# An expert stage of 25 planned tiles: idle tiles placed as second tiles of the first experts

## The reference

```
attn = softmax(window-64 causal scores of q, k) @ v          # (4, 8, 576, 64)
x = attn as (2304, 512)
h = x @ w_in ; g = h - tanh(h) ; x = g @ w_out              # d_ff 2048
logits = unit(x) @ unit(expert_emb).T / tau                  # 8 experts
expert_idx = argmax(logits) ; gate_w = softmax(logits) at it
for e in range(8):                                           # w1[e] 512 x 1024, w2[e] 1024 x 512
    mask = expert_idx == e
    out[mask] = gate_w[mask, None] * (maximum(x[mask] @ w1[e], 0) @ w2[e])
```

## Time and profile before

| | |
|---|---|
| median of 3 runs | 871.54 us (871.42 to 874.31) |
| the profiled execution, its own time | 873.4 us |
| its span, first to last instruction | 871.6 us |
| TensorE busy in the span | 809.0 us (93%) |
| VectorE, ScalarE, GpSimd | 478.6, 360.3, 218.6 us |
| mean granted clock of TensorE | 0.967 |
| matmuls with w1, with w2 in each of their three forms | 176, 176 |
| gathers and scatters of tiles | 25, 25 |

### The profile page before, as it was taken

The page is one execution under the profiler, slowest core; times in us unless marked ns, Lnnn a source line. Parts: engine busy times, 40 slices in busy tenths (PEclk is TensorE's granted clock), DMA queues, the critical chain, the costliest instruction groups (busy, mean ns, idle before and its releaser), DMA issues. The chain is left out here.

```text
span 871.6 us, 16504 instructions
## 1 busy us (share of the span) xinstructions
PE 809.0 (93%) x4604; PEld 689.5 (79%) x4605; DVE 478.6 (55%) x1421; ACT 360.3 (41%) x880; POOL 218.6 (25%) x284
## 2 busy tenths in 40 slices
PE   6699999999999999999999999399999999999992
PEld 5588888888888888888888998277888888888871
DVE  7356655775577557755774575555534252545422
ACT  4444554333433343334332223416544253655423
POOL 4647542223222322231223001221111111111111
PEclk9699999999999999999999999679999999999996
DMA  9862113331322133313216120126452342565110
GB/s 176 243 202 64 45 37 97 74 71 36 96 71 72 37 93 75 73 37 97 55 38 211 51 65 1 39 83 235 170 198 83 132 143 73 199 228 218 51 40 22
DMA packets 106310, 87.87 MB, mean 101 GB/s; under 512 B 79012, under 2 KB 80169, under 8 KB 106242
## 3 DMA queue, kind: packets, MB, share of 16 engines
q1 hardware_dynamic: 98386, 74.92, 29.4%
q0 software_dynamic: 4624, 11.32, 4.2%
q10 hardware_dynamic: 3232, 0.79, 0.5%
HBM read 152.87 MB, written 11.46 MB: 189 GB/s over the span
## 5 line engine op out<-in xcount | busy, mean ns | idle before, releaser
L1233 PE MATMUL banks<-xh,win_h 128*128 128x384 f32 x384 | 137.8, 359 | 2.1 <-POOL xl L529 2.1
L1235 PE MATMUL banks<-xh,win_l 128*128 128x384 f32 x384 | 130.8, 341 | 0.0
L1234 PE MATMUL banks<-xl,win_h 128*128 128x384 f32 x384 | 130.5, 340 | 0.0
L701 ACT ACTIVATE gf<-banks 128x384 f32<-128x384 f32 x96 | 47.1, 491 | 183.0 <-PE banks L1235 182.9
L519 POOL TENSOR_TENSOR sm<-sm,rr 128x384 f32<-128x384 f32 x48 | 50.6, 1055 | 275.8 <-DVE rr L872 275.8
L1233 PE MATMUL banks<-wout_h,gh 128*128 128x512 f32 x288 | 118.8, 413 | 0.0
L1235 PE MATMUL banks<-wout_h,gl 128*128 128x512 f32 x288 | 113.7, 395 | 0.0
L1234 PE MATMUL banks<-wout_l,gh 128*128 128x512 f32 x288 | 113.2, 393 | 0.0
L933 DVE TENSOR_TENSOR gl<-gf,gh 128x384 fp32r<-128x384 f32 x96 | 55.0, 573 | 104.2 <-ACT gh L708 104.2
L708 ACT CAST gh<-gf 128x384 fp32r<-128x384 f32 x96 | 49.1, 512 | 129.5 <-PE banks L1235 128.3
L929 DVE TENSOR_TENSOR gf<-banks,gf 128x384 f32<-128x384 f32 x96 | 53.2, 554 | 69.6 <-ACT gf L701 68.5
(11 more groups left out here) (186 smaller groups left out, 1537.8 us busy)
## 6 DMA issues: line engine op xcount, KB each, us to landing
w1raw<-in_moe_w_dram SPq DMA_DIRECT2D x104, 512.0 KB
w2raw<-in_moe_w_dram SPq DMA_DIRECT2D x104, 512.0 KB
x2T<-unit_embeddings SPq DMA_DIRECT2D x20, 256.0 KB, 3.4
junk<-unit_embeddings SPq DMA_DIRECT2D x20, 256.0 KB, 3.5
x_rows<-x SPq DMA_DIRECT2D x6, 768.0 KB, 6.3
wout_raw<-in_moe_w_out_dram SPq DMA_DIRECT2D x4, 1024.0 KB, 7.7
win_raw<-in_moe_w_in_dram SPq DMA_DIRECT2D x3, 1024.0 KB, 10.1
vw<-in_v_dram SPq DMA_DIRECT2D x16, 192.0 KB, 3.4
```

Source lines behind the costliest of these rows:

```text
L701: act.activation(gf[c % 2][:], psH[c % 2], ACT.Tanh).then_inc(tanh_ready, 1)
L1233: pe.matmul(to, sh, mh, start=start, stop=False)
L1234: pe.matmul(to, sh, ml, start=False, stop=False)
L1235: return pe.matmul(to, sl, mh, start=False, stop=stop)
```

## The change

The plan is computed anew. It counts the tiles that are left over (`idle_tiles` = 25 less the sum of `tiles`), and marks as many experts from the first on (`left_over`, by comparing the expert's number, `em8` + 8, with that count). Each marked expert is `given` one tile more. `ends`, `starts` and the openings are computed from `given`. Within a marked expert the second tile is the idle one: its row in the table lies behind the expert's filled rows, and the tiles behind it move down by one (`local`, `second`, `third`). `rows` is now found for each tile by the expert whose stretch it lies in (`shown`). `is_idle` is one for the second tile of each marked expert that has tokens, and `plan[:, 3]` is one less it. So with three tiles left over, experts 0, 1 and 2 have an idle second tile, and no tile is idle behind the last expert.

The program of the four engines after the plan is the same, instruction for instruction, apart from the banks: `psY` is 4 and 5, `psXG` is 6.

```diff
--- before.py
+++ after.py
@@ -202,6 +202,10 @@
         experts_ended = sb("experts_ended", [P, NTILE], scope=phase2)
         row = [sb(f"row{i}", [P, 1], scope=phase2) for i in range(2)]
         rows = sb("rows", [P, 1], I32, phase2)
+        idle_tiles = sb("idle_tiles", [P, 1], scope=phase2)
+        total = sb("total", [P, 1], scope=phase2)
+        is_idle = sb("is_idle", [P, NTILE], scope=phase2)
+        d8 = [sb(f"d8_{i}", [P, E], scope=phase2) for i in range(12)]
 
         mstep, dstep = sem("mstep"), sem("dstep")
         ident_made, masks_made, pads_zeroed, consts_made = sem("ident_made"), sem("masks_made"), sem("pads_zeroed"), sem("consts_made")
@@ -270,8 +274,8 @@
         psJ = banks[:, 0, :]
         psG = [banks[:, i, :] for i in (0, 1)]
         psHT = [banks[:, i, :] for i in (2, 3)]
-        psY = [banks[:, i, :] for i in (4, 6)]
-        psXG = banks[:, 5, :]
+        psY = [banks[:, i, :] for i in (4, 5)]
+        psXG = banks[:, 6, :]
 
         q_blocks, k_blocks = (x.rearrange("b h (i p) d -> p (b h i) d", p=WINDOW) for x in (q, k))
         win_rows = w_in.rearrange("(k p) f -> p k f", p=P)
@@ -1058,29 +1062,52 @@
             then(dve.tensor_copy(count, psN))
             then(dve.tensor_tensor(cmp18[:], count.unsqueeze(2).broadcast_to((P, E, MAXT)), tiles18[:], ALU.is_gt))
             then(dve.tensor_reduce(tiles, cmp18[:], AX, ALU.add))
-            then(dve.tensor_tensor(prod8[:], tiles.unsqueeze(1).broadcast_to((P, E, E)), tri8[:], ALU.mult))
+            left_over, given, shown, later, second, third, local, base = (t[:] for t in d8[:8])
+            then(dve.tensor_reduce(total[:], tiles, AX, ALU.add))
+            then(dve.tensor_scalar(idle_tiles[:], total[:], -1.0, float(NTILE), ALU.mult, ALU.add))
+            then(dve.tensor_scalar(left_over, em8[:, 0, :], float(E), idle_tiles[:, 0:1], ALU.add, ALU.is_lt))
+            then(dve.tensor_tensor(given, tiles, left_over, ALU.add))
+            then(dve.tensor_tensor(prod8[:], given.unsqueeze(1).broadcast_to((P, E, E)), tri8[:], ALU.mult))
             then(dve.tensor_reduce(ends, prod8[:], AX, ALU.add))
-            then(dve.tensor_scalar(moves, tiles, -float(P), float(REGION), ALU.mult, ALU.add))
-            then(dve.tensor_scalar(passed, ends, pcol[:, 0:1], None, ALU.is_le))
-            then(dve.tensor_tensor(jumped, passed, moves, ALU.mult))
+            then(dve.tensor_tensor(starts, ends, given, ALU.subtract))
+            then(dve.tensor_scalar(local, starts, -1.0, pcol[:, 0:1], ALU.mult, ALU.add))
+            then(dve.tensor_scalar(second, local, 1.0, None, ALU.is_equal))
+            then(dve.tensor_scalar(third, local, 2.0, None, ALU.is_ge))
+            then(dve.tensor_scalar(base, tiles, -1.0, None, ALU.add))
+            then(dve.tensor_tensor(second, second, base, ALU.mult))
+            then(dve.tensor_tensor(second, second, third, ALU.subtract))
+            then(dve.tensor_tensor(second, second, left_over, ALU.mult))
+            then(dve.tensor_tensor(local, local, second, ALU.add))
+            then(dve.scalar_tensor_tensor(out=base, in0=rowbase[:, 0, :], scalar=1.0 / P, in1=local, op0=ALU.mult, op1=ALU.add))
+            then(dve.tensor_scalar(passed, ends, pcol[:, 0:1], None, ALU.is_gt))
+            then(dve.tensor_scalar(later, starts, pcol[:, 0:1], None, ALU.is_gt))
+            then(dve.tensor_tensor(shown, passed, later, ALU.subtract))
+            then(dve.tensor_tensor(jumped, shown, base, ALU.mult))
             then(dve.tensor_reduce(row[0][:], jumped, AX, ALU.add))
-            then(dve.tensor_scalar(row[1][:], row[0][:], 1.0 / P, pcol[:, 0:1], ALU.mult, ALU.add))
-            dve.tensor_scalar(rows[:], row[1][:], float(E * REGION // P), None, ALU.min).then_inc(rows_planned, 1)
+            dve.tensor_scalar(rows[:], row[0][:], float(E * REGION // P), None, ALU.min).then_inc(rows_planned, 1)
 
 
             then(dve.tensor_tensor(ended[:], jcol[:].unsqueeze(2).broadcast_to((P, NTILE, E)), ends.unsqueeze(1).broadcast_to((P, NTILE, E)), ALU.is_ge))
             then(dve.tensor_reduce(experts_ended[:], ended[:], AX, ALU.add))
             then(dve.tensor_scalar(plan[:, 0, :], experts_ended[:], float(E - 1), None, ALU.min))
-            then(dve.tensor_tensor(starts, ends, tiles, ALU.subtract))
-            then(dve.scalar_tensor_tensor(out=filled, in0=tiles, scalar=0.0, in1=notfirst[:], op0=ALU.is_gt, op1=ALU.mult))
+            then(dve.scalar_tensor_tensor(out=filled, in0=given, scalar=0.0, in1=notfirst[:], op0=ALU.is_gt, op1=ALU.mult))
             then(dve.tensor_tensor(ended[:], jcol[:].unsqueeze(2).broadcast_to((P, NTILE, E)), starts.unsqueeze(1).broadcast_to((P, NTILE, E)), ALU.is_ge))
             then(dve.tensor_tensor(moved[:], ended[:], filled.unsqueeze(1).broadcast_to((P, NTILE, E)), ALU.mult))
             then(dve.tensor_reduce(changes[:, 1:NTILE + 1], moved[:], AX, ALU.add))
+            then(dve.scalar_tensor_tensor(out=later, in0=tiles, scalar=0.0, in1=left_over, op0=ALU.is_gt, op1=ALU.mult))
+            then(dve.tensor_scalar(starts, starts, 1.0, None, ALU.add))
+            then(dve.tensor_tensor(ended[:], jcol[:].unsqueeze(2).broadcast_to((P, NTILE, E)), starts.unsqueeze(1).broadcast_to((P, NTILE, E)), ALU.is_equal))
+            then(dve.tensor_tensor(moved[:], ended[:], later.unsqueeze(1).broadcast_to((P, NTILE, E)), ALU.mult))
+            then(dve.tensor_reduce(is_idle[:], moved[:], AX, ALU.add))
             then(dve.tensor_tensor(plan[:, 1, :], changes[:, 1:NTILE + 1], changes[:, 0:NTILE], ALU.subtract))
             then(dve.tensor_copy(plan[:, 2, :], changes[:, 1:NTILE + 1]))
             then(dve.tensor_scalar(plan[:, 2, :], plan[:, 2, :], 1, None, ALU.bitwise_and))
-            then(dve.tensor_scalar(plan[:, 3, :], jcol[:], ends[:, E - 1:E], None, ALU.is_lt))
+            then(dve.tensor_scalar(plan[:, 3, :], is_idle[:], -1.0, 1.0, ALU.mult, ALU.add))
             dve.sem_inc(planned, 1)
             low_first_w1([0])
 
```

## The result

| | before | after |
|---|---|---|
| median of the runs | 872.01 us (4 runs) | 883.45 us (4 runs, 881.06 to 885.14) |
| ratio | 1 | 1.0124, 95% interval 1.0094 to 1.0155 |
| the profiled execution, its own time and span | 873.4, 871.6 us | 885.1, 883.3 us |

The change makes the kernel 1.2% slower, 11.4 us. The forecast was 872.9 us in a range of 869.3 to 878.5, so it was wrong, by 10.6 us. The step that failed is the clock of TensorE: the forecast's sum put nothing for a fall of the clock in the new pauses, and it fell three times, for 5.7 us. Waits in the same sum were also too short, by 5.0 us together, of which Part 3 had foreseen 0.6.

A forecast was written before the change was run, and what follows sets the result against it. TensorE was taken as the bound, busy 230 of 230 us at full clock through the middle of the expert stage. Terms -12.3 + 3.7 + 5.3 + 3.7 + 0.6 + 0.4 = +1.4 us gave 872.9 us, range 869.3 to 878.5.

The forecast's parts named there:

- Part 3: Weight fetches: w1 pieces for experts 1 and 2 land late, 0.3 us each, 0.6 us cost in all.
- Part 1: End of the program: idle tiles no longer follow the last real tile, and its step transposes no tokens; gain 12.3 us.
- Part 4: Plan: 18 more VectorE operations delay the copy of the token numbers and the first gather; cost 0.4 us.
- Part 5: Banks: token transposes and second products swap banks 5 and 6; nothing either way.
- these lie between what held and what fell: New TensorE pauses, 4.2 us in steps 2 and 5, 3.4 in step 1, against earlier pauses that kept or lost the clock.
- Rival A: TensorE's clock falls in the new waits; two falls of 2.2 us give 877.3 us; chance 0.15.
- Part 2: Idle tiles inside the expert stage take cover away: cost 3.7 us at expert 2, 5.3 at expert 1, 3.7 at expert 0.
- rival B: Weight fetches for the next expert: w1 pieces land 2 to 3 us later than taken in both experts, 877 us; chance 0.10.

The follow-up runs named there:

- the experiment: The kernel before with the change's banks and 18 more small plan operations, idle tiles still at the end: 872.35 us against 872.28, ratio 1.0007.
- the kernel with both edits: The changed kernel with filler matmuls in TensorE's idle-tile skips and half the bytes of w1 for experts 1 to 7: 877.12 us, ratio to before 1.0047.

## Why the prediction was wrong

**What held.** The bound and the structure: 22 runs of each kind, TensorE the bound, steps of 12.3 us outside the affected ones. Part 1: 12.3 us forecast, 11.9 at the end plus 0.5 in the last step (11.01 us from its w1 run to its hidden transposes, 11.51 in the others). Part 4: 0.4 us forecast, 0.34 by the trace, 0.2 to 0.3 in the experiment, under what runs can tell. Part 5: nothing, as forecast. The transposes of step 2, held by the casts ahead of relu, came 7.63 us behind the w1 run; 7.57 was forecast. The pause behind them was 4.2 us, as forecast, with the casts back to back.

**What failed.** The forecast's own case assumed that the clock holds, so its sum has no term for a fall. It gave that the sentence "these lie between what held and what fell" and then a chance of 0.15 to its falling. It fell in or just behind all three long pauses of the change, and cost 5.7 us in the runs themselves. The pause of 4.2 us ahead of the w1 run of tile 3 came out as forecast, and the clock fell behind it all the same. Rival A had the mechanism right and a price of 4.4 us for two falls, 2.2 each; the three cost 2.4, 1.6 and 1.6. The third is in step 1, whose pause between products was not 3.4 but 5.3 us; that 3.4 us would have held is doubtful, since a pause of 3.4 us lost the clock in the kernel with both edits. The account that rival A names from the Trainium skill ("TensorE: Matmul & The Clock Gate", HAM oscillation) describes what happened: a wait behind a burst, and a cold start of the next. The trace agrees for the three pauses of 4.2 us and more, with a granted clock of 0.50 in the run behind each, and not for those of 2.2 to 2.8 us in the same trace, which kept 1.00. I had two held pauses of a little over 2 us and one fall, 5.7 us behind the last products, to go by, and two pauses of 4.2 us between them; to take the favourable side there was a choice, not a reading.

**What was mis-sized in Part 2.** Three terms, with the change's own profile:

| term | forecast | measured | more by |
|---|---|---|---|
| step 1, token transposes to w2 run | 0.36 us | 1.83 | 1.5 |
| step 5, w1 run to hidden transposes | 7.6 (Part 3 had 0.3 beside it) | 9.5 | 2.0 |
| the other pauses around idle tiles, each 0 to 0.4 us longer | | | 1.5 together |

The first is TensorE's restart. I took 0.36 us from a step in which it goes straight on. Here it had waited for the gather, and 0.92 us of idle time stand ahead of the run, ended by nothing but "issue". That these are the flag reads and the branch, which run ahead unseen where TensorE has other work, is my reading; no run takes them away. Some 1.9 us stand there too behind the late gather of the kernels that give expert 2 its idle second tile (634.51 to 636.42 and 635.87 to 637.79 above), though the profile puts the end of that wait down to VectorE. The second is 1.24 us of late w1 and 0.74 us ahead of the casts, as read from the run with half of w1. Part 3 had worked out the fetch for tile 3 alone and taken the same 0.3 us for tile 6. For tile 3 SyncE asked when forecast (588.5 for 588.7) and nothing was late; for tile 6 it asked 4 us later against the step. Why it did is not shown. The third is the same kind of thing in small: 2.27 to 2.57 us where 2.17 stood, 2.67 where 2.34 stood.

**The ledger.** Part 2 had 12.8 us before rounding. With 5.7 for the clock, 1.5 for the restart in step 1, 2.0 for step 5 and 1.5 for the other pauses these are the 23.4 us measured (12.76 + 5.67 + 1.47 + 1.97 + 1.52). Of the 10.6 us beyond Part 2 the forecast had 0.6, as Part 3.

**The chances.** Rival A came true, with one fall more than it had, and rival B in part: 1.24 us at one of the two experts, where it had 2 to 3 us at both. They came in one run. That a late weight itself loses the clock is not shown: with half of w1 the pause ahead of tile 6 was 5.1 us without late weights, and the clock fell there too. The range ended at 878.5 us because I added the rivals as alternatives. A joint case with both and the restarts was not in it.

## What to carry to other kernels

A tile without work is not free where the pipeline is full: it takes away the matmuls that hid the casts, the flag reads and the transfers of its neighbours, and here cost 4.2 to 6.2 us inside, without the clock, against 4 us at the end (11.9 us for three). Skip it on every engine rather than move it. When a change opens pauses on TensorE, ask for the longest one and whether the clock has held over one as long in the same trace; if it hasn't, count on the fall and price it from the slow rows, and put late inputs on top of it, since both can come in one run.

## What the runs showed of the hardware

- The granted clock fell in, or up to 1.3 us behind, every pause between products of 3.2 us or more that the traces have inside the expert stage (3.2, 3.4, 4.2, 4.7, 5.3 and 6.4 us among them), though each of them held eight transposes or more. It held over those of 2.3 to 3.1 us. A fall cost 1.6 to 2.9 us in the run behind it.
- Matmuls that nobody reads, put into the skips, kept the clock up in the two places where the pause that was left is 2.3 to 2.4 us: the w2 run of tile 0 went from 8.0 to 5.6 us.
- Behind a wait for a gather, TensorE took 1.8 us from four token transposes to the next matmul, with two flag reads and a branch between; in a normal step the same code takes 0.36 us.
- Reading the flags of some ten branches on GpSimd at the end took about 4 us more than keeping them in registers, by one profile of each (15.1 and 11.2 us from the last scatter to the end).
